# Weight staging, last shifts and the first tile's normalisation re-ordered at the seam between attention and the channel MLP

## The reference

```python
def reference(q, k, v, ...):            # B, H, S, D = 4, 8, 576, 64
    attn_out = _attn_ref(q, k, v)       # sliding window of 128, slopes as bias, softmax
    x = attn_out.transpose(0, 2, 1, 3).reshape(B, S, H * D)     # 4 x 576 x 512
    # mixer and MLP
    mixed = np.real(np.fft.fft(np.fft.fft(x, axis=1), axis=2))
    u = x + mixed
    un = (u - mean(u)) / np.sqrt(var(u) + 1e-6)
    x = u + np.maximum(un @ w_ch1, 0.0) @ w_ch2                 # 512 -> 2048 -> 512
    # routed experts: expert e per token by argmax or by the token before, gated by a local gate
    out[b, s] = p[e] * (np.maximum(x[b, s] @ w1[e], 0.0) @ w2[e])
```

## Time and profile before

| | us |
|---|---|
| median of 3 runs | 900.96 |
| the three runs | 900.43, 900.96, 906.88 |
| the profiled execution, its own time | 899.51 |
| its span in the profile | 897.6 |
| TensorE busy | 844.9 (94% of the span) |
| VectorE, ScalarE, GpSimd busy | 548.0, 307.4, 272.2 |

### The profile page before, as it was taken

One profiled execution on the slowest core, in us unless ns is written; L12 is line 12 of the kernel. 1 busy time (PEld: TensorE's weight loads), 2 busy tenths in 40 slices (PEclk: granted clock), 3 DMA queues, 4 the chain that ended last, 5 costly groups with the idle time before them and its releaser, 6 DMA issues.

```text
span 897.6 us, 22524 instructions
## 1 busy us (share of the span) xinstructions
PE 844.9 (94%) x8820; PEld 607.7 (68%) x8821; DVE 548.0 (61%) x1125; ACT 307.4 (34%) x461; POOL 272.2 (30%) x287
## 2 busy tenths in 40 slices
PE   8988988799999999999999999939999999999995
PEld 4776777776667676767676767517777777777773
DVE  6899987866757474748483839769995883000000
ACT  5789887543111111111111111103333333333331
POOL 1457878311010101011111100013444444334431
PEclk9999999999999999999999999959999999999998
DMA  9455543458110101010101003405774772111100
GB/s 289 133 176 159 175 144 98 134 184 236 48 48 23 47 23 47 23 47 23 47 23 47 24 24 133 126 27 165 259 236 143 229 234 77 48 45 50 50 24 0
DMA packets 60474, 91.28 MB, mean 102 GB/s; under 512 B 7304, under 2 KB 30971, under 8 KB 60421
## 3 DMA queue, kind: packets, MB, share of 16 engines
q1 hardware_dynamic: 55061, 74.80, 26.9%
q0 software_dynamic: 5360, 15.74, 5.5%
...
## 4 chain that ended last, share of the span: by engine, by line
PE 70%; DVE 11%; DMA 7%; SPq 3%; issue 3%; ACT 3%; POOL 1%; DVEq 0%; POOLq 0%; ACTq 0%
PE psum L926 19%; PE psum L909 19%; PE psum L1102 13%; PE psum L1086 13%; DMA m_mem<-in_qk 2%; DVE arena L1436 1%; DVE m_mem L1408 1%; DMA arena<-in_mlp_w 1%; PE psum L1053 1%; SPq L627 1%; DMA m_mem<-x_rows,m_mem 1%; PE psum L676 1%; DVE arena L1429 1%; ACT psum L1161 1%; PE psum L885 1%
## 5 line engine op out<-in xcount | busy, mean ns | idle before, releaser
L909 PE MATMUL psum<-m_mem,arena 128*128 (+1 forms) x1728 | 197.6, 273 | 0.0
L926 PE MATMUL psum<-arena,m_mem 128*128 128x512 f16 x864 | 195.5, 379 | 0.4 <-DVE m_mem L1590 0.4
L909 PEld LDWEIGHTS psum<-m_mem,arena 128*128 128x128 f16 x1728 | 169.1, 98 | 27.8 <-issue 0.4
L926 PEld LDWEIGHTS psum<-arena,m_mem 128*128 128x128 f16 x864 | 84.5, 98 | 91.1 <-DVE m_mem L1590 0.9
L1086 PEld LDWEIGHTS psum<-m_mem,arena 128*128 x2400 | 137.1, 97 | 7.0 <-issue 1.5
L1086 PE MATMUL psum<-m_mem,arena 128*128 128x128 f16 x2400 | 139.5, 218 | 1.2 <-issue 0.6
L1102 PE MATMUL psum<-arena,m_mem 128*128 x600 | 133.4, 379 | 0.0
L1269 ACT ACTIVATE m_mem<-psum 128x512 f16<-128x512 f32 x72 | 43.0, 597 | 236.1 <-PE psum L909 236.1
L1619 DVE SCALAR_TENSOR_TENSOR m_mem<-m_mem,arena 128x512 f16<-128x512 f32 x144 | 102.8, 768 | 0.0
L1102 PEld LDWEIGHTS psum<-arena,m_mem 128*128 128x128 f16 x600 | 57.6, 98 | 65.2
L2001 POOL TENSOR_TENSOR arena<-m_mem,arena 128x1024 f16<-128x1024 f32 x9 | 19.2, 2138 | 255.1 <-ACT arena L1280 210.4
...
## 6 DMA issues: line engine op xcount, KB each, us to landing
...
```

The source lines that it names most:

```text
L909: last = nc.tensor.matmul(psum[:, 2 + k % 4, (f % 2) * 2 * P:(f % 2 + 1) * 2 * P], w1_sb[:, sp_, c, f * P:(f + 1) * P], unT[:, bass.ds(t % ...
L926: last = nc.tensor.matmul(psum[:, 6 + q, :], hT[:, k % 4, sp_, at:at + P], w2_sb[:, mp, f, :], start=f == 0 and sp_ == 0 and mp == 0, stop ...
```

## The change

The change touches only the seam and tile 0 of the MLP.

- SyncE: the last item's four shifts and its store come before the loads of chunks 4 and 5. Weight staging has ten buffers in place of four; the six new ones lie in the part of `arena` that attention used, so they are filled only behind the last item. The two first expert chunks are asked for ahead of the gate's columns, and the routing's nine tables behind them. The gate's columns are written over some of the new staging buffers, and so come when the last chunk is split.
- VectorE: `normalise(15)` comes before the splits of chunks 0 and 1. The first tile's `moments` and `normalise_u` come ahead of the middle rows and of the last two spectra.
- ScalarE: chunks 4 to 8 are cast later, two fewer chunks before tile 0; `x_hi_of` of the two last items comes earlier, `copy_b` behind both.
- GpSimd makes the low parts of the two last items, in place of VectorE.

```diff
-W_DFT = 7
-W_TILE0 = [3, 3, 4, 3, 4, 4, 0, 0]
+W_DFT = 5
+W_TILE0 = [4, 4, 4, 3, 4, 4, 0, 0]
...
         w_staging = [wstage[:, 0, :], wstage[:, 1, :], end_space[:, 0:CH], end_space[:, CH:2 * CH]]
+        W_EARLY = len(w_staging)
+        late_at = [ends_at + 2 * D - 2 * P] + [SLOT_WORDS - 2 * CH * (i + 1) for i in range(5)]
+        w_staging += [arena[:, at:at + 2 * CH].bitcast(F32) for at in late_at]
         WRING = len(w_staging)
...
             shift_x(PAIRS - 2)
             store_x(PAIRS - 2)
-            W_TOP = W_SPEC + W_DFT
-            for n in range(WRING, WRING + 2):
-                load_w(n)
             shift_x(PAIRS - 1)
             store_x(PAIRS - 1)
+            for n in range(W_EARLY, W_EARLY + 3):
+                load_w(n)
...
-            for n in range(WRING + 2, W_TOP + 3):
+            for n in range(W_EARLY + 3, WRING + 9):
                 load_w(n)
...
-            load_w(W_TOP + 3)
             sp.wait_ge(edge_rows, 2)
             sp.dma_start(x_dram[B * SP_ROWS:B * SP_ROWS + B, :], x288[0:B, :]).then_inc(edge_stored, 16)
-            for dst, src in ((prefix_sb, prefix), (ids_sb, ids), (iota_sb, iota_e), (negiota_sb, neg_iota),
-                             (reset_sb, reset), (thr_sb, thresholds), (slot_iota, slotiota), (blk_iota, blkiota)):
-                sp.dma_start(dst, src).then_inc(tables_in, 16)
-            sp.dma_start(kiota_sb[0:1], kiota).then_inc(tables_in, 16)
...
             sp.dma_start(gate_dram, gateT).then_inc(gate_out, 16)
-            for n in range(W_TOP + 4, WCH):
+            for n in range(WRING + 9, WCH):
                 load_w(n)
+            load_exp(0)
+            load_exp(1)
             sp.wait_ge(gate_out, 16)
             for e in range(E + 1):
                 sp.dma_start(gate_cols[e].rearrange("p (c j) -> p c j", c=DC),
...
-            load_exp(0)
-            load_exp(1)
+            for dst, src in ((prefix_sb, prefix), (ids_sb, ids), (iota_sb, iota_e), (negiota_sb, neg_iota),
+                             (reset_sb, reset), (thr_sb, thresholds), (slot_iota, slotiota), (blk_iota, blkiota)):
+                sp.dma_start(dst, src).then_inc(tables_in, 16)
+            sp.dma_start(kiota_sb[0:1], kiota).then_inc(tables_in, 16)
...
@@ scalar
             spectrum_hi(0, (1,))
-            w_hi_of(4)
             x_hi_of(PAIRS - 3)
             middle_hi_of(1)
             spectrum_hi(1, (0,))
-            w_hi_of(5)
             xl_hi_of(B - 1)
+            x_hi_of(PAIRS - 2)
             spectrum_hi(1, (1,))
             act.wait_ge(m_clear, 1)
+            x_hi_of(PAIRS - 1)
             copy_b(0, first=True, at=4)
-            x_hi_of(PAIRS - 2)
+            w_hi_of(4)
+            spectrum_hi(2, (0,))
+            w_hi_of(5)
+            spectrum_hi(2, (1,))
             w_hi_of(6)
-            x_hi_of(PAIRS - 1)
-            spectrum_hi(2, (0,))
+            std_of(0)
+            spectrum_hi(3, (0,))
+            middle_hi_of(2)
+            spectrum_hi(3, (1,))
             w_hi_of(7)
-            spectrum_hi(2, (1,))
+            unT_hi_of(0, at=4)
             w_hi_of(8)
-            middle_hi_of(2)
-            spectrum_hi(3, (0,))
-            w_hi_of(9)
-            std_of(0)
-            spectrum_hi(3, (1,))
-            unT_hi_of(0, at=4)
-            w_hi_of(10)
@@ vector
             normalise(PAIRS - 2)
-            for n in range(W_SPEC // 2):
-                w_lo_of(n)
             normalise(PAIRS - 1)
...
             spectrum_lo(0)
+            w_lo_of(0)
+            w_lo_of(1)
             dve.wait_ge(middle_clear, 1)
             middle_lo_of(1)
-            w_lo_of(2)
...
-            w_lo_of(3)
-            w_lo_of(4)
+            w_lo_of(2)
             spectrum_lo(1, (1,))
             end_fold_d(PAIRS - 1)
             fold(0, first=True, at=4)
+            w_lo_of(3)
+            spectrum_lo(2, (0,))
+            w_lo_of(4)
+            spectrum_lo(2, (1,))
+            moments(0)
             w_lo_of(5)
-            spectrum_lo(2, (0,))
-            end_x_lo(PAIRS - 2)
-            w_lo_of(6)
-            spectrum_lo(2, (1,))
-            end_x_lo(PAIRS - 1)
-            w_lo_of(7)
-            moments(0)
+            normalise_u(0, un_first)
+            spectrum_lo(3, (0,))
             middle_lo_of(2)
-            w_lo_of(8)
-            spectrum_lo(3, (0,))
-            normalise_u(0, un_first)
-            w_lo_of(9)
             spectrum_lo(3, (1,))
             unT_lo_of(0, at=4)
-            w_lo_of(10)
+            for n in range(6, 9):
+                w_lo_of(n)
@@ gpsimd, behind the gather of the first tile's rows
+            x_lo_of(PAIRS - 2)
+            x_lo_of(PAIRS - 1)
```

8 lines of the change are left out of this document (1 added, 7 removed).

## The result

| | median, us | runs | lowest, highest |
|---|---|---|---|
| before, in the same series | 903.03 | 19 | 900.43, 906.88 |
| after | 898.16 | 19 | 892.31, 901.19 |

The ratio is 0.9942, 95% interval 0.9928 to 0.9957: 5.2 us faster (3.9 to 6.5), within 1%, where 6.9 were forecast. The absolute 894.0 was 4.2 too low: 2.1 of this is before itself, 903.03 here and 900.96 in the three runs shown, and the rest is the forecast's own. 898.16 lies just above the top of the range, 898.0; the ratio times 900.96 gives 895.7, inside it.

What follows compares the result with a forecast made beforehand. TensorE's idle time and clock were taken as the bound: 7.5 us of waits gone plus 2.6 of clock, less 3.2 of new waits, net 6.9; 892.6 from the profiled 899.51, 894.0 as median, range 891.0 to 898.0.

Steps and rivals of the forecast that it cites:

- The waits that go: TensorE, seam and tile 0: six waits of before vanish, 7.5 us together.
- The new wait at the gate's transpose: TensorE waits for work moved behind `normalise_u`: 2.4 us, bounds 1.5 and 3.
- The seventh spectrum's wait: TensorE ahead of the seventh spectrum: a new wait of 0.7 us, bounds 0 and 1.9.
- the walk: Seam stepped through on the times of before; put the seventh spectrum's new wait at 0.5 us.
- The clock: TensorE from the first transposes through the edge: full clock stays, 2.6 us gained, bounds 0 and 2.6.
- the clock falls all the same: Rival, chance 0.18: clock falls around the gate's wait and thin edge, costing 2.6 us, perhaps 3; 897.0 us.
- Normalisation of item 15: VectorE at the seam: without two splits ahead it ends at 152.1, so TensorE's 0.66 us wait goes.
- Last shifts: SyncE, item 15: issued 1.2 us earlier, landing after 1.8 to 3.7 us; the 0.49 us wait goes.
- Tile 0: Ten buffers and later tables bring chunks in time: waits of 1.50 and 0.41 us go, bounds 0 and 1.9.
- the ring does not help: Rival, chance 0.07: staging is held otherwise, so tile 0's 1.50 and 0.41 us waits stay; 895.9 us.
- The better packing: Rival, chance 0.10: ScalarE and VectorE pack better at the seam, new waits 1.0 us, 9.1 gained; 891.8 us.
- The slower rival: Chance 0.04: VectorE stands for all 6.5 us of GpSimd's work between 160 and 170 us; 901.9 us.

Runs made afterwards that it cites:

- n1_splits_first: Changed kernel with VectorE's splits of chunks 0 and 1 between the last two normalisations again; 897.51 us, ratio to before 0.994.
- r1_after_again: Changed kernel profiled and timed once more with no edit; 897.68 us, ratio to before 0.9941.
- e1_ring_of_four: Changed kernel with four weight staging buffers instead of ten, loads up to chunk 12 ahead of the edge's rows; 901.59 us, ratio to before 0.9985.

## Why the prediction was right, and where not

**The waits that go: right, all six.** 0.66, 0.49, 0.72, 3.73, 1.50 and 0.41 have no row in after but the 0.19. For the 0.49 this is in part luck: at the same place, the fourth spectrum's low part, four of the changed kernel's variants waited 1.17 to 1.43 us when the last shift landed late. The new wait at the gate's transpose was forecast as 2.4 and is 2.48, the one at the first transposes as 0.1 and is 0.19.

**The seventh spectrum's wait: the right chain, the wrong size.** The step "0.7, near the walk's 0.5, since only the fold and the splits are exposed" failed; it is 1.75 to 1.98. The walk had `end_fold_d(15)` at its free duration, though it too has two inputs in SBUF. What the forecast worked out from the Trainium skill (SBUF — State Buffer, Who interferes with whom) was 1.9, and the page's rule, that such an instruction and one of GpSimd that reads SBUF hold the shared port each for its whole length, agrees with the 0.7 us by which the fold always ends behind GpSimd's. My argument against it was that few instructions were exposed; one on the chain was enough. That 1.9 and 1.75 are so close is partly chance: it has a whole low part of 1.40 us as the hold, and the hold measured here is 0.9. Counted from the start of the seam, the fifth spectrum's low part was ready 1.0 us later than my walk had it, and TensorE arrived 0.2 us earlier.

**The clock: wrong.** "I take it that the clock stays" failed in after and in the second profile of it. The rival "the clock falls all the same" happened, at 1.5 us where it had 2.6 to 3: here the clock fell at 184.5, inside the edge, and in before at 176.1, so that the transposes and the whole edge ran at the lower level. My grounds were that the clock stood for 2.9 us after the last matmul in before and that waits of 1.24 and 1.50 did no harm. Of the eight gate waits of 2.41 to 2.49 us in these profiles all eight were followed by a fall.

**Normalisation of item 15: the effect, and half of the reason.** I priced the order; `n1_splits_first` shows that the splits at their old place cost TensorE nothing there where GpSimd does not hold them.

**Last shifts: mostly unproven.** Counted from the start of the seam, the issue is 0.95 us earlier in after (+5.97 for +6.92) and 0.8 in `r1_after_again`, where 1.2 was forecast. The landing "after 1.8 to 3.7 us" was 1.8 in after, but up to 4.1 elsewhere. I had connected the 3.7 with the two loads in flight; the three late landings without loads ahead show that it also comes without them.

**Tile 0: right.** 1.91 us of waits gone; it is 46.55 before and 45.15 after, 1.40 less: the low clock takes 0.9 more there, and 0.4 are of the rest. The rival "the ring does not help" is refuted by `e1_ring_of_four`: without the ring nearly the whole gain is gone.

**The better packing** did not come: the new waits are 4.4 us where that rival had 1.0. **The slower rival** needed VectorE to stand for all of GpSimd's work; `normalise_u` would have to end later than 177.3 on the clock of before, +28.4, and ended at +24.0.

In sum: forecast 7.5 - 3.2 of waits and 2.6 of clock; found 3.1 of waits, 1.2 of clock, and 0.6 of rest that no step had. The waits were 1.2 too good, nearly all at the seventh spectrum, the clock 1.4, and the rest made up for 0.6, which is luck. The range had no good ground: "at their best 10 us, at their worst about 2" does not follow from the bounds of the steps. They give 7.5 + 2.6 - 1.5 = 8.6 at best, and at worst 7.5 - 1.9 of waits that go less 1.9 + 0.8 + 3 of new ones, which is nothing gained: about 892 to 901. The signs of what would show it did their work: "granted clock near 0.5 before that up-projection" and "splits over 1.5 us between 160 and 170" were named as refutations, and both came (0.50 at 185; 1.88 us for the second of the two splits at 161.25, and 1.69 for the fold).
